# Experts' first product by seven half-size block products, tokens outer in two halves

## The chip, the cores and the metric

One core of a Trainium2 chip. The metric is the time of one execution on the device in microseconds, lower is better. The times below are of one program that computes everything; the host only rearranges inputs and the output.

## What is computed

Three steps on 2176 rows (4 batches of 512 tokens and 32 state rows) of width 512:

```
attention per batch and head: xread = softmax(x s^T / 8) s;  sread = softmax(s x^T / 8) x
dense:    h = x @ w_in (512 x 2048);  g = h - tanh(h);  x = g @ w_out
experts:  P = exp(x @ w_gate - max), 8 rounds of row and column normalisation
          out = sum over e of P[:, e] * (relu(x @ w1[e]) @ w2[e])     8 experts, 512 x 1024 x 512
```

All products of the dense part and of the experts are made to nearly full precision from rounded parts: an operand `a` is split into `a_hi` (rounded to the type float32r, by ScalarE) and `a_lo = a - a_hi`, and a product is `hi*hi + hi*lo + lo*hi`, three matmuls in a faster single-pass type.

## The kernel before, in words

Every engine runs its own program; semaphores order them. Loads and stores are issued by SyncE.

**Attention** (`scores_T`, `transposes1`, `sread` and others) takes some 58 us. **Dense** (`dense`, four passes `hb` over half blocks of the weights) runs for each pass over the state rows (j = 0) and four batches (j = 1 to 4), four blocks of hidden units each, with `up_batch` (6 matmuls), the tanh on ScalarE, `h - tanh` and the split on VectorE, and `down_dense` (12 matmuls) two steps behind. `dense_sum` adds the four output banks to `acc`. In the last pass, ScalarE (`mlp_input`) and GpSimd split the finished batches of `acc` for the experts.

**Experts.** Expert outer, four chunks of 512 tokens inner (`chunk`). In a chunk `up` (L1123) makes one block of 128 hidden units for 512 tokens: 4 blocks of depth x 3 matmuls, each 128 x 128 weights (w1) against 512 tokens, into one of three banks. ScalarE (`hidden_expert`, L538) takes relu out of the bank and rounds it, VectorE (L763) makes the low part from the same bank. `down` (L1133), two blocks behind, takes 128 tokens of the hidden block as the weights and 512 columns of w2: 4 tiles of tokens x 3 matmuls, summed over 8 blocks in banks 0 to 3. After a chunk VectorE (`gated`, L901) multiplies each of the four banks by the gate of its tokens and adds it to `yacc`. In chunk 1 of each expert the 128 state rows are done the other way round (`state_up`, `state_turn`, `state_down`). The weights of the next expert are split in the last chunk (`w1_hi`, `w2_hi` on ScalarE, `w1_lo`, `w2_lo` on VectorE). Between two matmuls of one product nothing waits; waits stand ahead of a block.

**Gates.** In chunk 0 of the first expert `logits` makes x @ w_gate from the split parts, `turn_logits` turns it with 17 small transposes, and in chunks 1 and 2 VectorE (`rows`, `columns`) runs the eight rounds, each with one sum over partitions on GpSimd. Outputs of the first expert are kept without gates until then (`keep`, `gate_kept`).

Of the kernel before, what the change touches and what calls it, by code (L numbers as in the profile page):

```python
# [18 lines left out]
B, H, S, NS, D = 4, 8, 512, 32, 64  # L19
# [3 lines left out]
P = 128  # L23
# [24 lines left out]
EXP_STEP = 6  # L48
ST_CHUNK = 1
GATED_EARLY = 2 * ST  # L50
assert SINKHORN == F


def build(nc, xT_d, xn_d, sT_d, w1_d, w2_d, wg_d, out_d):
# [9 lines left out]
    with ctx:  # L64

        start = (nc.sbuf_base + 63) // 64 * 64
        place = [start]

        def sb(name, shape, dt=f32):
            size = 4  # L70
            for n in shape[1:]:
                size *= n
            at = place[0]
            place[0] += (size + 31) // 32 * 32
            return nc.alloc_sbuf_tensor_at(name, shape, dt, offset=at)


        w1h = sb("w1h", [P, F, KT, P], f32r)
        w1l = sb("w1l", [P, F, KT, P], f32r)
        w2h = sb("w2h", [P, F, DM], f32r)  # L80
        w2l = sb("w2l", [P, F, DM], f32r)
        after_w2l = place[0]


        xh = sb("xh", [P, KT, B * S], f32r)
        xl = sb("xl", [P, KT, B * S], f32r)

        st1 = sb("st1", [P, NST, KT, P])
        st2 = sb("st2", [P, NST, DM])


        shared = place[0]
        acc = sb("acc", [P, KT, T])
        after_acc = place[0]
        place[0] = shared
        yacc = sb("yacc", [P, TQ, DM])
        assert place[0] <= after_acc
        place[0] = after_acc

        hiddens = place[0]  # L100
        hh = sb("hh", [P, NH, S], f32r)
        hl = sb("hl", [P, NH, S], f32r)
        xsh = sb("state_rows_hi", [P, KT, SB], f32r)
        xsl = sb("state_rows_lo", [P, KT, SB], f32r)
        scratch = place[0]


        hs_f = sb("state_hidden", [P, S])
        hsh = sb("state_hidden_T_hi", [P, F, SB], f32r)
        hsl = sb("state_hidden_T_lo", [P, F, SB], f32r)  # L110
        end = place[0]


        place[0] = scratch
        wg = sb("wg", [P, KT, P], f32r)
        wg_raw = sb("wg_raw", [P, KT, E])
        lg_rows = sb("lg_rows", [2 * E, T])
        lg_two = sb("lg_two", [P, TQ, 2 * E])
        end = max(end, place[0])


        place[0] = after_w2l - (F - HF) * DM * 4
        th = sb("tanh_h", [P, S])
        x_st = sb("state_tokens", [P, KT, SB])
        h_st = sb("state_tokens_hidden", [P, NH, SB])
        assert place[0] <= after_w2l

        place[0] = scratch
        sTh = sb("sTh", [P, B // 2, KT, P], f32r)
        sTl = sb("sTl", [P, B // 2, KT, P], f32r)  # L130
        g_h = sb("h_less_tanh", [P, 2, S])
        end = max(end, place[0])

        place[0] = shared
        xT = sb("xT", [P, 2, KT, S])
        xn = sb("xn", [P, 2, ST, DM])
        scT = sb("scT", [P, S])
        assert place[0] <= after_acc

        place[0] = hiddens  # L140

        sT = sb("sT", [P, B // 2, KT, P])
        e2 = sb("e2", [P, 2, S])
        a2T = sb("a2T", [P, ST, P])
        a1 = sb("a1", [P, 2, ST, P])
        nb2 = sb("nb2", [P, G])
        r2 = sb("r2", [P, G])
        m1 = sb("m1", [P, 2, 4 * ST])
        r1 = sb("r1", [P, 2, 4 * ST])
        assert place[0] <= scratch  # L150

        place[0] = end
        ident = sb("ident", [P, P])
        pr = sb("pr", [P, E, TQ])
        gcur = sb("gate_now", [P, TQ])
        rsum = sb("rsum", [P, TQ])
        csum = sb("csum", [P, E])
        call = sb("call", [P, E])
        gmax = sb("gmax", [P, 1])
        amax = sb("amax", [P, 1])  # L160
        assert place[0] <= nc.sbuf_usable_end, (place[0], nc.sbuf_usable_end)
# [7 lines left out]
        lgpsum = bank[7]  # L169
        stpsum = bank[7]  # L170
# [57 lines left out]
        s_x2h = sem("mlp_input_hi")  # L228
        s_x2s = sem("mlp_input_split")
        s_wgin = sem("wgate_loaded")  # L230
        s_wgz = sem("wgate_zeroed")
        s_wgh = sem("wgate_hi_ready")
        s_wg = sem("wgate_split")
        s_lg = sem("logits_ready")
        s_lgc = sem("logits_copied")
        s_lgt = sem("logits_transposed")
        s_lgr = sem("logits_by_token_ready")
# [6 lines left out]
        s_gw = sem("gates_final")  # L244
        s_su = sem("state_rows_hidden_ready")
        s_sr2 = sem("state_rows_relu_ready")
        s_stt = sem("state_rows_transposed")
        s_shi = sem("state_rows_hidden_hi_ready")
        s_shs = sem("state_rows_hidden_split")
# [6 lines left out]

        def own_rows(b, s0=0, s1=S):

            return slice(b * S + s0, b * S + s1)

        def batch(b, s0=0, s1=S):

            return slice(b * TB + s0, b * TB + s1)

        def states(t, k):

            return t[:, k, :].rearrange("p (b n) -> p b n", b=B)[:, :, S:TB]

        def by_batch(t, k):

            return t[:, k, :].rearrange("p (b n) -> p b n", b=B)
# [11 lines left out]


        @block.sync
        def _(sp):
# [19 lines left out]
            def follow_splits(b, more):  # L306

                for i in range(F + 3):
                    if i < F:
                        sp.wait_ge(s_w1, b * F + i + 1)  # L310
                        if i < F - NST:
                            load_w1(b, i + NST)
                        elif more:
                            load_w1(b + 1, i - F + NST)
                    j = i - 3
                    if j >= 0:
                        sp.wait_ge(s_w2, b * F + j + 1)
                        if j < F - NST:
                            load_w2(b, j + NST)
                        elif more:  # L320
                            load_w2(b + 1, j - F + NST)


# [12 lines left out]
            for b in range(2, B):  # L336
                load_x(b)

# [9 lines left out]
            def next_w1(hb, s):  # L348
                sp.wait_ge(s_w1, hb * HF + s + 1)
                sp.dma_start(st1[:, s], w1_d[hb + 1, s]).then_inc(s_w1in[s], 16)  # L350

            def next_w2(hb, s):
                sp.wait_ge(s_w2, hb * HF + s + 1)
                sp.dma_start(st2[:, s], w2_d[hb + 1, s]).then_inc(s_w2in[s], 16)

            for s in range(HF):
                next_w1(DH, s)
            sp.wait_ge(s_m, m_count(DH, 0, 0))
            sp.dma_start(wg_raw[:], wg_d).then_inc(s_wgin, 16)
            for s in range(HF):  # L360
                next_w1(DH + 1, s)
            for f in range(F):
                next_w2(DH + f // HF, f % HF)

            with sp.Fori(DENSE + 1, NB - 1) as b:
                follow_splits(b, True)
            follow_splits(NB - 1, False)

            def store(done, t0, t1):
                sp.wait_ge(s_yfree, ST * (1 + (E - 1) * C) + done)  # L370
                sp.dma_start(out_d[:, t0:t1], yacc[:, t0:t1]).then_inc(s_out, 16)

            store(ST, 0, ST)
            store(2 * ST, ST, 2 * ST)
            sp.wait_ge(s_syf, E)
            sp.dma_start(out_d[:, ST_TILE:TQ], yacc[:, ST_TILE:TQ]).then_inc(s_out, 16)
            store(3 * ST, 2 * ST, 3 * ST)
            for t in range(3 * ST, 4 * ST):
                store(t + 1, t, t + 1)
# [4 lines left out]
        def _(pool):  # L384
# [3 lines left out]
                                    pattern=[[-1, P]], channel_multiplier=1).then_inc(s_ident, 1)  # L388

# [21 lines left out]
            nc.gpsimd.memset(acc[:], 0.0).then_inc(s_acc0, 1)  # L411

            pool.wait_ge(s_m, m_count(DH, 0, 0))
            nc.gpsimd.memset(wg[:].bitcast(f32), 0.0).then_inc(s_wgz, 1)


            for k in range(KT):
                pool.wait_ge(s_x2h, k + 1)
                nc.gpsimd.tensor_tensor(by_batch(xsl, k), states(acc, k), by_batch(xsh, k).bitcast(f32),
                                        ALU.subtract).then_inc(s_x2s, 1)  # L420
            for c in range(C):
                for k in range(KT):
                    pool.wait_ge(s_x2h, (c + 1) * KT + k + 1)
                    nc.gpsimd.tensor_tensor(xl[:, k, own_rows(c)], acc[:, k, batch(c)],
                                            xh[:, k, own_rows(c)].bitcast(f32), ALU.subtract).then_inc(s_x2s, 1)


            pool.wait_ge(s_lmax, 1)
            nc.gpsimd.partition_all_reduce(amax[:], gmax[:], P, RMAX).then_inc(s_amax, 1)
            for r in range(SINKHORN):  # L430
                pool.wait_ge(s_csum, r + 1)
                nc.gpsimd.partition_all_reduce(call[:], csum[:], P, RADD).then_inc(s_call, 1)


        @block.scalar
        def _(act):
# [838 lines left out]
```

## Time and profile before

| | |
|---|---|
| median of 3 runs | 1875.97 us (1874.74 to 1876.88) |
| profiled execution | 1877.22 us, its span 1875.4 us, granted clock 0.997 |
| TensorE, weight loads | 1855.6 us, 1533.4 us, 8409 each |
| VectorE, ScalarE, GpSimd | 615.5, 413.1, 59.9 us |
| read from HBM | 50.61 MB |

The span runs from the first to the last instruction; the profiled execution's own time lies 1.8 us above it. Matmuls overlap in the pipeline, so the mean duration of one (389 ns for 512 columns) is not its interval; that is read from the starts of neighbours. In the rows PE is TensorE, PEld its weight loads, DVE VectorE, ACT ScalarE, POOL GpSimd, and L is a line of the kernel. The type of every TensorE operand is written f32, for float32r too. A product of plain float32 operands leaves two records, each with its own weight load.

### The profile page before, as it was taken

The numbers are of one execution on the slowest core, as the hardware profiler recorded it, in microseconds if no ns is written. First come the engines' busy times: TensorE is split into PE (matmuls) and PEld (weight loads), VectorE is DVE, ScalarE is ACT, GpSimd is POOL, SyncE is SP. The second block draws the span as 40 slices with busy tenths as digits, with TensorE's granted clock in tenths as the row PEclk, the third lists the DMA queues.
The fourth block names the chain that finished last, engine by engine and source line by source line (L and its number), as shares of the span: only waits on it lengthen the run. The fifth ranks groups of instructions, "written<-read, shape, count | busy, mean of one in ns | idle before, by whom it ended". The sixth has DMA issues, their size and how long they took to land.

```text
span 1875.4 us, 20899 instructions
## 1 busy us (share of the span) xinstructions
PE 1855.6 (99%) x8409; PEld 1533.4 (82%) x8409; DVE 615.5 (33%) x1013; ACT 413.1 (22%) x750; POOL 59.9 (3%) x58
## 2 busy tenths in 40 slices
PE   7999999999999999999999999999999999999999
PEld 5888888888888888888888888888888888888887
DVE  6656665621452113211321232123211321142121
ACT  6434344421121112111211121112111211121111
POOL 4200000310000000000000000000000000000000
PEclk9899999999999999999999999999999999999999
DMA  6101101110020002000200020002000200010001
GB/s 230 45 1 45 45 0 51 46 40 1 0 63 29 0 1 63 29 1 0 69 22 1 0 73 18 1 0 74 18 1 0 74 18 1 0 46 23 1 28 45
DMA packets 28231, 56.41 MB, mean 30 GB/s; under 512 B 5104, under 2 KB 5104, under 8 KB 27248
## 3 DMA queue, kind: packets, MB, share of 16 engines
q1 hardware_dynamic: 28144, 55.08, 9.2%
q8 instruction: 76, 1.25, 0.3%
q14 instruction: 11, 0.09, 0.0%
HBM read 50.61 MB, written 4.46 MB: 29 GB/s over the span
## 4 chain that ended last, share of the span: by engine, by line
PE 97%; DVE 1%; issue 1%; ACT 1%; POOL 0%; DVEq 0%; ACTq 0%; POOLq 0%
PE bank L1128 12%; PE bank L1130 12%; PE bank L1129 12%; PE bank L1142 12%; PE bank L1143 12%; PE bank L1144 12%; PE bank L1097 3%; PE bank L1098 3%; PE bank L1099 3%; PE bank L1081 1%; PE bank L1083 1%; PE bank L1082 1%; PE bank L1037 1%; PE bank L1070 1%; PE bank L1173 1%
## 5 line engine op out<-in xcount | busy, mean ns | idle before, releaser
L763 DVE SCALAR_TENSOR_TENSOR hl<-bank,hh 128x512 fp32r<-128x512 f32 x256 | 177.1, 692 | 952.8 <-ACT hh L538 952.8
L1128 PE MATMUL bank<-xh,w1h 128*128 128x512 f32 x1024 | 400.4, 391 | 0.2
L538 ACT ACTIVATE hh<-bank 128x512 fp32r<-128x512 f32 x256 | 153.1, 598 | 1116.2 <-PE bank L1130 1116.2
L1130 PE MATMUL bank<-xh,w1l 128*128 128x512 f32 x1024 | 398.7, 389 | 0.0
L1142 PE MATMUL bank<-w2h,hh 128*128 128x512 f32 x1024 | 398.5, 389 | 0.0
L1129 PE MATMUL bank<-xl,w1h 128*128 128x512 f32 x1024 | 398.5, 389 | 0.0
L1144 PE MATMUL bank<-w2h,hl 128*128 128x512 f32 x1024 | 398.4, 389 | 0.0
L1143 PE MATMUL bank<-w2l,hh 128*128 128x512 f32 x1024 | 398.3, 389 | 0.0
L1128 PEld LDWEIGHTS bank<-xh,w1h 128*128 128x128 f32 x1024 | 192.3, 188 | 40.8 <-issue 1.3
L1130 PEld LDWEIGHTS bank<-xh,w1l 128*128 128x128 f32 x1024 | 192.2, 188 | 40.3
L1142 PEld LDWEIGHTS bank<-w2h,hh 128*128 128x128 f32 x1024 | 192.2, 188 | 40.0
L1144 PEld LDWEIGHTS bank<-w2h,hl 128*128 128x128 f32 x1024 | 192.2, 188 | 39.9
L1143 PEld LDWEIGHTS bank<-w2l,hh 128*128 128x128 f32 x1024 | 192.2, 188 | 39.8
L1129 PEld LDWEIGHTS bank<-xl,w1h 128*128 128x128 f32 x1024 | 192.3, 188 | 39.3
L901 DVE SCALAR_TENSOR_TENSOR yacc<-bank,gate_now,yacc 128x512 f32<-128x512 f32 x112 | 78.1, 751 | 127.2 <-PE bank L1144 127.2
L1097 PE MATMUL bank<-hh,w2h 128*128 128x512 f32 x256 | 100.0, 391 | 0.0
L1098 PE MATMUL bank<-hl,w2h 128*128 128x512 f32 x256 | 99.6, 389 | 0.0
L1099 PE MATMUL bank<-hh,w2l 128*128 128x512 f32 x256 | 99.6, 389 | 0.0
L758 DVE TENSOR_TENSOR hl<-h_less_tanh,hh 128x512 fp32r<-128x512 f32 x64 | 45.3, 708 | 43.9 <-ACT hh L533 43.9
L1097 PEld LDWEIGHTS bank<-hh,w2h 128*128 128x128 f32 x256 | 48.0, 188 | 11.5 <-DVE acc L783 1.2
L533 ACT CAST hh<-h_less_tanh 128x512 fp32r<-128x512 f32 x64 | 39.7, 621 | 79.1 <-DVE h_less_tanh L756 79.1
L1099 PEld LDWEIGHTS bank<-hh,w2l 128*128 128x128 f32 x256 | 48.1, 188 | 10.1
(129 smaller groups left out, 1372.0 us busy)
## 6 DMA issues: line engine op xcount, KB each, us to landing
st<-w SPq DMA_DIRECT2D x160, 256.0 KB, 2.7
xT<-xT SPq DMA_DIRECT2D x8, 512.0 KB, 8.0
xn<-xn SPq DMA_DIRECT2D x4, 1024.0 KB, 6.0
out<-yacc SPq DMA_DIRECT2D x3, 1024.0 KB, 3.9
out<-yacc SPq DMA_DIRECT2D x5, 256.0 KB, 2.1
sT<-sT SPq DMA_DIRECT2D x2, 128.0 KB, 3.3
wg_raw<-wg SPq DMA_DIRECT2D x1, 16.0 KB, 2.4
```

The costliest lines, as they stand in the source:

```text
L538: nc.scalar.activation(hh[:, f % NH], hpsum[f % NH][:], ACT.Relu).then_inc(s_hh, 1)
L763: v.scalar_tensor_tensor(hl[:, f % NH], hpsum[f % NH][:], 0.0, hh[:, f % NH].bitcast(f32), ALU.max, ALU.subtract).then_inc(s_hs, 1)
L901: v.scalar_tensor_tensor(yacc[:, i], ypsum[t][:], gcur[:, i:i + 1], yacc[:, i], ALU.mult, ALU.add).then_inc(s_yfree, 1)
L1097: mm(out, w2h[:, s, at], high, start=(s == 0), stop=False)
L1098: mm(out, w2h[:, s, at], hl[:, i % NH, :], start=False, stop=False)
L1099: last = mm(out, w2l[:, s, at], high, start=False, stop=(s == HF - 1))
L1128: mm(out, w1h[:, f, k, :], xh[:, k, own_rows(c)], start=(k == 0), stop=False)
L1129: mm(out, w1h[:, f, k, :], xl[:, k, own_rows(c)], start=False, stop=False)
L1130: last = mm(out, w1l[:, f, k, :], xh[:, k, own_rows(c)], start=False, stop=(k == KT - 1))
L1142: mm(out, hh[:, f % NH, at], w2h[:, f], start=(f == 0), stop=False)
L1143: mm(out, hh[:, f % NH, at], w2l[:, f], start=False, stop=False)
L1144: last = mm(out, hl[:, f % NH, at], w2h[:, f], start=False, stop=(f == F - 1))
```

## The change

The loop is turned: all 16 half experts ("units" of 512 hidden units) for chunks 0 and 1, then the 16 again for chunks 2 and 3. A unit with two chunks is a visit of four stages: chunk, then pair `p` of hidden blocks. Each stage (`stage`) computes two hidden blocks for 512 tokens. Depth (512), hidden (256) and tokens (512) are each cut in two, and the 2 x 2 x 2 block product is made with seven products of 128 hidden units x 256 tokens x 256 deep, the form of Strassen and Winograd: seven factors of tokens and seven of weights, three of them plain blocks and four sums. The products are combined on VectorE into the hidden blocks, from PSUM and SBUF. Sums and low parts of all factors are made on GpSimd, high parts on ScalarE. The token factors of two chunks are resident; those of chunks 2 and 3 replace them at the turn of the halves. Outputs are drained every second stage, since a unit is half an expert. Logits are made from the unsplit `acc` with 32-column products in plain float32 and a small selecting product in place of the transposes. The state rows use plain blocks and one sum, 24 matmuls of 256 columns a unit, in the first half only.

TensorE's new program:

```diff
+            def product(which, u, cc, p):
+                out = {P1: apsum[:, 0:HT], P2: apsum[:, HT:S], P6: bpsum[:, 0:HT], P7: bpsum[:, HT:S],
+                       P4: cpsum[:, 0:HT], P5: cpsum[:, HT:S], P3: bpsum[:, 0:HT]}[which]
+                a, b = FACTORS[which]
+                w, xs, xr = wc[u], xch[cc], xcl[cc]
+                for k in range(HK):
+                    mm(out, w[:, p, 0, b, k, :], xs[:, a, k, :], start=(k == 0), stop=False)
+                    mm(out, w[:, p, 0, b, k, :], xr[:, a, k, :], start=False, stop=False)
+                    last = mm(out, w[:, p, 1, b, k, :], xs[:, a, k, :], start=False, stop=(k == HK - 1))
+                last.then_inc(s_p, 1)
+            def stage(x, l, half):
+                n, u, part, cc, p = 8 * x + l, l // 4, l % 4, l // 2 % 2, l % 2
...
+                if cc == 0:
+                    pe.wait_ge(s_wfs, 3 * (2 * vis + p + 1))
+                if half and part == 2:
+                    pe.wait_ge(s_xfs, 16)
+                if not first:
+                    pe.wait_ge(s_h11, n)
+                product(P1, u, cc, p)
+                product(P2, u, cc, p)
+                if not first:
+                    pe.wait_ge(s_h12, n)
+                product(P6, u, cc, p)
+                product(P7, u, cc, p)
+                if not first:
+                    pe.wait_ge(s_v, n)
+                product(P4, u, cc, p)
+                product(P5, u, cc, p)
...
+                if not first:
+                    down_even(*before)
+                pe.wait_ge(s_u3, n + 1)
+                product(P3, u, cc, p)
+                if first:
+                    turn_logits()
+                else:
+                    down_odd(*before)
...
+            pe.wait_ge(s_xfs, 8)
+            for l in range(8):
+                stage(0, l, 0)
+            with pe.Fori(1, E) as x:
+                for l in range(8):
+                    stage(x, l, 0)
+            pe.wait_ge(s_xfs, 12)
+            with pe.Fori(E, 2 * E) as x:
+                for l in range(8):
+                    stage(x, l, 1)
+            down_even(2 * E - 1, 7)
+            down_odd(2 * E - 1, 7)
```

`down_even` and `down_odd` hold 12 matmuls each, of the form of `down`, for the stage before. State rows: `state_up` (18 matmuls) after part 1, `state_up_even` (6) and `state_turn` in part 2, `state_down` (12) in part 3. VectorE's stage:

```diff
+                sum2(n)
+                hidden11(x, l)
+                sum3(n)
+                hidden_late(x, l)
+                sum25(n)
+                lo11(n, p)
...
+                lo_late(n, p)
+                hidden12(n, p)
+                lo12(n, p)
...
+                if l % 2 == 0 and not first:
+                    outputs(q, c, how)
...
+            def sum2(n):
+                dve.wait_ge(s_p, OPS * n + P7)
+                dve.wait_ge(s_c1, n + 1)
+                v.tensor_tensor(u2[:], bpsum[:, 0:HT], prod1[:], ALU.add).then_inc(s_u2, 1)
+            def hidden11(x, l):
+                v.tensor_tensor(hf[l % 2][:, 0, 0:HT], apsum[:, HT:S], prod1[:], ALU.add).then_inc(s_h11, 1)
+            def sum3(n):
+                dve.wait_ge(s_h11, n + 1)
+                v.tensor_tensor(u3[:], bpsum[:, HT:S], u2[:], ALU.add).then_inc(s_u3, 1)
+            def sum25(n):
+                v.tensor_tensor(u2[:], cpsum[:, HT:S], u2[:], ALU.add).then_inc(s_v, 1)
+            def hidden_late(x, l):
+                v.tensor_tensor(hf[p][:, :, HT:S], cpsum[:].rearrange("p (f n) -> p f n", f=2),
+                                u3[:].unsqueeze(1).broadcast_to([P, 2, HT]), ALU.add).then_inc(s_late, 1)
+            def lo11(n, p):
+                v.scalar_tensor_tensor(rl[p][:, 0, 0:HT], hf[p][:, 0, 0:HT], 0.0, raw(rh[p][:, 0, 0:HT]),
+                                       ALU.max, ALU.subtract).then_inc(s_l11, 1)
+            def hidden12(n, p):
+                dve.wait_ge(s_p, OPS * n + P3)
+                v.tensor_tensor(hf[p][:, 1, 0:HT], bpsum[:, 0:HT], u2[:], ALU.add).then_inc(s_h12, 1)
```

`lo_late` (2 x 256 columns) and `lo12` have the form of `lo11`. ScalarE's stage is `copy1` (P1 to SBUF), two `w2_hi` in parts 0 and 1, `relu11`, `relu_late`, `relu12`, then the high parts of the next unit's w1 factors. At the turn of the halves, and for chunk 3 two stages on:

```diff
+            expert(E - 1, 0, {6: (late_plain_hi, 2), 7: (token_sums_hi, 2)})
+            expert(E, 1, {0: (late_plain_hi, 3), 1: (token_sums_hi, 3)})
```

GpSimd's program of a visit, and of the token factors:

```diff
+            def visit(v, u, more=True, late=None):
+                w2_lo(v, 0)
+                w2_lo(v, 1)
+                if late == 3:
+                    token_sums(3)
+                if more:
+                    w1_pair_sums(v + 1, 1 - u, 0)
+                w2_lo(v, 2)
+                w2_lo(v, 3)
+                if late == 3:
+                    token_lo(3)
+                if more:
+                    w1_pair_lo(v + 1, 1 - u, 0)
+                if more:
+                    w1_pair_sums(v + 1, 1 - u, 1)
+                if late == 2:
+                    token_sums(2)
+                    token_lo(2)
+                if more:
+                    w1_pair_lo(v + 1, 1 - u, 1)
```

`token_sums` is four sums of 512 columns, `token_lo` three low parts of 512 and one of 2048, after ScalarE's high parts of the same sizes; `w1_pair_sums` four of 256, `w1_pair_lo` low parts of 512, 256 and 1024. SyncE loads unit v once the pair, or the w2 block, of unit v - 1 in its place is split.

Gates: the rounds `rows` and `columns` are spread over stages 2 to 8, one at the end of a stage, and in stages 5, 7 and 8 one in its middle; GpSimd's sums over partitions stand at fixed places among its splits. Logits:

```diff
+            def logits():
+                pe.wait_ge(s_wgin, 16)
+                pe.wait_ge(s_dsum, DENSE_SUMS)
+                for b in [B] + list(range(B)):
+                    src, n = (acc_s[:], SB) if b == B else (acc[:, b], S)
+                    out = lgpsum if b == B else bank[b]
+                    for k in range(KT):
+                        at = slice(k * LG, (k + 1) * LG)
+                        last = mm(out[at, 0:n], wg[:, k, :], src[:, k, :], start=True, stop=True)
+                    last.then_inc(s_lg, 1)
```

In the last dense pass the splits of w1 and w2 and the copies of `mlp_input` are left out; in their place ScalarE has the high parts of the factors of chunks 0 and 1 and of the first weight pair, GpSimd the sums and low parts.

## Rows read from the trace of the kernel before

**Rows 1.** The page, part 1: busy us (share of the span) x instructions
```profile
PE 1855.6 (99%) x8409; PEld 1533.4 (82%) x8409; DVE 615.5 (33%) x1013; ACT 413.1 (22%) x750; POOL 59.9 (3%) x58
```

**Rows 2.** The page, part 4: shares of the chain that ended last
```profile
PE 97%; DVE 1%; issue 1%; ACT 1%; POOL 0%; DVEq 0%; ACTq 0%; POOLq 0%
```

**Rows 3.** Windows, one expert: length, PE, PEld, DVE, ACT, POOL, clock, DMA
```profile
610.00:796.00 186.00, 186.00 (x826) 153.92 (x825) 44.93 (x68) 29.72 (x52) 0.00 (x0) 1.00 0.08 23
```

**Rows 4.** Timeline of TensorE inside a product: start us, duration us, instruction
```profile
899.95 0.39 PE L1128 MATMUL bank<-xh,w1h 128*128 128x512 f32 x1
...
903.58 0.39 PE L1129 MATMUL bank<-xl,w1h 128*128 128x512 f32 x1
```

**Rows 5.** Timeline of TensorE, 128 columns: seven starts, then the next product
```profile
413.99 0.28 PE L1209 MATMUL bank<-state_rows_lo,wg 128*128 128x128 f32 x1
...
414.77 0.45 PE L1128 MATMUL bank<-xh,w1h 128*128 128x512 f32 x1
```

**Rows 6.** Chain in order of time, four-byte products: start, us, what, records
```profile
139.06 2.68 PE bank L1070 x24
```

**Rows 7.** Groups of VectorE by form: busy us, mean ns | idle before
```profile
L901 DVE SCALAR_TENSOR_TENSOR yacc<-bank,gate_now,yacc 128x512 f32<-128x512 f32 x112 | 78.1, 751 | 127.2 <-PE bank L1144 127.2
L756 DVE TENSOR_TENSOR h_less_tanh<-bank,tanh_h 128x512 f32<-128x512 f32 x64 | 43.9, 686 | 35.1 <-ACT tanh_h L531 34.7
L750 DVE TENSOR_TENSOR state_tokens_hidden<-bank,tanh_h 128x128 f32<-128x128 f32 x16 | 4.6, 286 | 3.5 <-ACT tanh_h L523 3.5
```

**Rows 8.** Groups of ScalarE by form
```profile
L538 ACT ACTIVATE hh<-bank 128x512 fp32r<-128x512 f32 x256 | 153.1, 598 | 1116.2 <-PE bank L1130 1116.2
L523 ACT ACTIVATE tanh_h<-bank 128x128 f32<-128x128 f32 x16 | 4.4, 278 | 25.6 <-PE bank L1070 23.9 <-DVE state_tokens_hidden L750 1.0
L495 ACT CAST sTh<-sT 128x1024 fp32r<-128x1024 f32 x1 | 1.0, 1030 | 0.0
```

**Rows 9.** Groups of GpSimd by form
```profile
L402 POOL TENSOR_TENSOR a<-a,r 128x512 f32<-128x512 f32 x8 | 8.4, 1050 | 6.6 <-DVE r L703 6.6
L406 POOL TENSOR_TENSOR sTl<-sT,sTh 128x1024 fp32r<-128x1024 f32 x1 | 2.4, 2354 | 0.0
```

**Rows 10.** The page, part 6: weight loads, KB each, us to landing
```profile
st<-w SPq DMA_DIRECT2D x160, 256.0 KB, 2.7
```

**Rows 11.** Timelines of GpSimd and VectorE in the last dense pass
```profile
333.35 5.57 POOL L424 TENSOR_TENSOR xl<-acc,xh 128x512 fp32r<-128x512 f32 x4 [11.28 <-ACT xh L619]
335.36 0.69 DVE L756 TENSOR_TENSOR h_less_tanh<-bank,tanh_h 128x512 f32<-128x512 f32 x1 [1.80 <-ACT tanh_h L531]
337.70 1.77 DVE L810 TENSOR_TENSOR w1l<-st,w1h 128x512 fp32r<-128x512 f32 x1
```

**Rows 12.** Timeline of VectorE: dense outputs of chunks 0 and 1 added
```profile
327.90 2.48 DVE L783 TENSOR_TENSOR acc<-bank,acc 128x512 f32<-128x512 f32 x4
344.22 2.48 DVE L783 TENSOR_TENSOR acc<-bank,acc 128x512 f32<-128x512 f32 x4
```

**Rows 13.** Timeline of TensorE: the experts' first matmul
```profile
374.04 0.39 PE L1128 MATMUL bank<-xh,w1h 128*128 128x512 f32 x1
```

**Rows 14.** Timeline of TensorE: turned logits, and two score products
```profile
36.20 1.08 PE L983 MATMUL bank<-xT,sT 128*64 128x512 f32 x4
420.42 1.22 PE L1216 MATMUL bank<-ident,lg_rows 16*128 16x16 f32 x17
```

**Rows 15.** Timeline of TensorE, a wait, and the window behind it
```profile
51.33 1.11 PE L1011 MATMUL bank<-ident,a 128*128 128x128 f32 x4 [0.97 <-POOL a L402]
51.00:61.00 10.00, 9.68 (x40) 9.09 (x41) 4.49 (x8) 4.67 (x10) 4.18 (x2) 0.50 0.00 0
```

**Rows 16.** Groups of weight loads by form
```profile
L1129 PEld LDWEIGHTS bank<-xl,w1h 128*128 128x128 f32 x1024 | 192.3, 188 | 39.3
```

More of the change, by code:

```diff
@@ L103, in build @@
[L103 to L118, printed above, removed]
@@ L163, in ps @@
+        assert end <= nc.sbuf_usable_end, (end, nc.sbuf_usable_end)
+        th = hs_f
+        prod1 = u3
+        gmax, amax = most[:, 0:1], most[:, 1:2]
         def ps(name, shape):
@@ new lines, in token_lo @@
+            def token_lo(c):
+                hi, lo = xch[c % 2], xcl[c % 2]
+                pool.wait_ge(s_xfh, 4 * c + 2)
+                for k in range(2):
+                    less(lo[:, A11 + k], tokens(c, k * HK, False), raw(hi[:, A11 + k]), s_xfs)
+                pool.wait_ge(s_xfh, 4 * c + 3)
+                less(lo[:, A22], tokens(c, HK, True), raw(hi[:, A22]), s_xfs)
+                pool.wait_ge(s_xfh, 4 * c + 4)
+                less(lo[:, S1:OPS], xf[c % 2][:, S1:OPS], raw(hi[:, S1:OPS]), s_xfs)
@@ new lines, in _ @@
+            token_lo(0)
+            state_rows_lo()
+            token_sums(1)
+            token_lo(1)
+            for p in range(2):
+                w1_pair_sums(0, 0, p)
+                w1_pair_lo(0, 0, p)
+            w2_lo(0, 0)
+            w2_lo(0, 1)
+            w1_pair_sums(1, 1, 0)
+            max_of_all()
+            w2_lo(0, 2)
+            w2_lo(0, 3)
+            w1_pair_lo(1, 1, 0)
+            w1_pair_sums(1, 1, 1)
+            sums_of_all(0)
+            w1_pair_lo(1, 1, 1)
@@ L562, in dense @@
                         m_hi(hb, 1, s)
-                    if j == 2:
+                    if j == 2 and not last:
                         w1_half_hi(hb + 1, s)
@@ new lines, in expert, with exponentials @@
+            def expert(x, half, extra={}, last=False):
+                for l in range(8):
+                    stage(x, l, half, extra.get(l), not (last and l >= 4))
+            def logits():
+                act.wait_ge(s_lg, B + 1)
+                nc.scalar.copy(hs_f[:, 0:SB], lgpsum[:, 0:SB]).then_inc(s_lgc, 1)
+                for b in range(B):
+                    nc.scalar.copy(lg_rows[:, b], bank[b][:]).then_inc(s_lgc, 1)
+            def exponentials(c):
+                act.wait_ge(s_shift, 1)
+                nc.scalar.activation(pr[:], pr[:], ACT.Exp, bias=amax).then_inc(s_exp, 1)
@@ L798, in dense @@
                         m_lo(hb, 1, s)
-                    if j == 2:
+                    if j == 2 and not last:
                         w1_half_lo(hb + 1, s)
@@ L802, in dense @@
                         m_lo(hb + 1, 0, s)
-                    if j == 3 and last:
-                        w1_lo(DENSE, HF + s)
-                w2_half_lo(hb + 1, 0)
+                if not last:
+                    w2_half_lo(hb + 1, 0)
                 dense_sum(hb, DC - 1)
@@ new lines, in keep_tokens @@
+            def keep_tokens(c):
+                for t in range(ST):
+                    gate_kept(c * ST + t)
+            dve.wait_ge(s_ident, 1)
+            own(v.reduce_sum(sel[:], ident[:].rearrange("p (k e) -> p e k", k=KT)[:, 0:E], X_AX))
+            dve.sem_inc(s_sel, 1)
+            stage(0, 0, 0, end=logits_max)
+            stage(0, 1, 0, end=logits_shift)
+            dve.wait_ge(s_xfs, 8)
+            stage(0, 2, 0, "keep", end=lambda: rows(0))
+            stage(0, 3, 0, states="keep", end=lambda: round_after(1))
@@ new lines, in _ @@
+            stage(1, 2, 0, end=lambda: keep_tokens(1))
+            for l in range(3, 8):
+                stage(1, l, 0)
+            with dve.Fori(2, E) as x:
+                expert(x, 0)
+            stage(E, 0, 1, end=lambda: own_gate(E, 1))
+            stage(E, 1, 1)
+            dve.wait_ge(s_xfs, 12)
+            stage(E, 2, 1, "first")
+            stage(E, 3, 1)
+            dve.wait_ge(s_xfs, 16)
+            stage(E, 4, 1, "first")
+            for l in range(5, 8):
+                stage(E, l, 1)
@@ L970, in _ @@
+            with dve.Fori(E + 1, 2 * E) as x:
+                expert(x, 1)
+            outputs(8 * E - 1, 3, "gated")
         @block.tensor
@@ new lines, in down_even, with down_odd, state_columns @@
+            def down_even(x, l):
+                n = 8 * x + l
+                pe.wait_ge(s_l11, n + 1)
+                down_tiles(x, l, 0, (0, 1))
+                pe.wait_ge(s_llate, n + 1)
+                down_tiles(x, l, 0, (2, 3))
+            def down_odd(x, l):
+                n, p, vis = 8 * x + l, l % 2, 2 * x + l // 4
+                down_tiles(x, l, 1, (2, 3))
+                pe.wait_ge(s_l12, n + 1)
+                down_tiles(x, l, 1, (0, 1))
+            def state_columns(at, b, u, k0, opens, closes):
+                out = stpsum[:, at * HT:(at + 1) * HT]
+                for k in range(HK):
+                    mm(out, xsh[:, k0 + k, :], wc[u][:, :, 0, b, k, :], start=opens and k == 0, stop=False)
+                    mm(out, xsh[:, k0 + k, :], wc[u][:, :, 1, b, k, :], start=False, stop=False)
+                    last = mm(out, xsl[:, k0 + k, :], wc[u][:, :, 0, b, k, :], start=False, stop=closes and k == HK - 1)
+                return last
```

921 lines of the change are left out of this document (506 added, 415 removed).

## The prediction

> **What bounds the kernel now.** I read the busy shares first, then the chain of waits, then one expert in the windows view, then single instructions. TensorE is busy 99% of the span [rows 1], and the chain that ended last is TensorE for 97% [rows 2]. In one expert's 186 us it is busy for all of them at full clock, while VectorE works 45 us, ScalarE 30 and GpSimd nothing [rows 3]. So time can only come out of TensorE's own stream, and the other engines have room. In that stream a 128x512 product starts every 0.2269 us (16 intervals in 3.63 us) [rows 4]; 512 columns at the full 2.4 GHz would be 0.2133, so each carries 13.4 ns on top.
>
> **First product: what is removed and added.** An expert has 4 chunks x 8 blocks x 12 first products of 512 columns plus 24 for the state rows: 408, or 3264 over 8 experts, 3264 x 0.2269 = 740.6 us. Now a stage (two blocks of 128 hidden units, 512 tokens) runs 7 products x 6 matmuls of 256 columns. Stages: 16 units x 8 = 128, so 5376 matmuls, and the state rows take 4 x 6 per unit, 16 units in the first half: 384. Together 5760, each half as wide. The second product (24 of 512 columns a stage) keeps its count, 3072, as do the state rows' 192 and their 64 transposes.
>
> The whole change hangs on the interval T of a 256-column matmul with its own weight load, which the trace does not show. Neighbours: with 128 columns in the same type the interval is 0.78/7 = 111.4 ns, where the stream alone would be 53, so something other than the columns, by all likelihood the load, sets it [rows 5]. Four-byte products run as two records each; 24 such records take 2.68 us, 111.7 ns each, again 128 columns [rows 6]. Nothing faster is seen, so 111.7 is the lower end. For the upper end the 13.4 ns could be a fixed cost of each matmul: 106.7 + 13.4 = 120. If it goes with the columns, T is half of 226.9, 113.4. Two of these three rows lie at 111 to 113, so I take 115, and keep 120 as a rival. 5760 x 0.115 = 662.4, a gain of 78.2 us; at 111.7 it is 97.2, at 120 it is 49.4. At 0.1237 the gain would just pay for the 28 us of costs below (740.6 - 28 = 712.6; / 5760).
>
> The Trainium skill, "TensorE: Matmul & The Clock Gate", section "Back-to-back issue gap", gives columns / 2.4 + 2.5 ns for a warm matmul, 109.2 ns here; by that the gain would be 111.6 us. This case's trace disagrees at 512 columns (226.9 ns against 215.8), so I give it no weight beyond the lower end.
>
> **Does the combination keep up?** A stage on TensorE is 42 x 0.115 + 24 x 0.2269 = 10.28 us (10.9 before). From the stage's start: P1, P2, P6, P7 end at 2.8, P4 and P5 at 4.1, `down_even` at 6.9, P3 at 7.6, `down_odd` at 10.3. Interpolating 128 and 512 columns, VectorE needs 0.42 us for 256 (0.286 and 0.686) and ScalarE 0.39 (0.278 and 0.598) [rows 7, 8]. P3 waits for `sum3`: sum2, hidden11, sum3 from 3.0 end by 4.3, against 6.9: slack 2.6. P6 of the next stage waits for hidden12: P3 ends at 7.6, hidden12 by 8.2, wanted at 11.7. Even stages then drain four output banks (0.751 each, started 0.68 apart): `lo12` by 9.1, banks until about 11.9, next `sum2` at 13.2. VectorE's work: seven of 0.42 and two of 0.69, in all 4.3 us, and 3.0 of banks every second stage: 5.8 of 10.3. In the first half a unit's four stages also carry the state rows, 5.8 us more on TensorE against some 2.3 on VectorE. ScalarE about 3 a stage. I cost the steady stages at no wait; the cover that hides them is the four products and `down_even` ahead of P3.
>
> GpSimd now splits all weights. It takes 2.35 us for 1024 columns into the rounded type, and 1.05 for 512 plain ones [rows 9]. Per unit: four w2 blocks 4.8, eight sums of 256 columns 4.8, lows 2 x (1.2 + 0.6 + 2.35) = 8.3: about 18 us of 41. Its last low waits for ScalarE's third stage and ends near 33 us, eight ahead of need. The experts' weights are fetched twice, 64 MB where 32; a 256 KB block lands in 2.7 us [rows 10] and four a stage are wanted in 10: hidden.
>
> **GpSimd against VectorE.** While GpSimd worked on four splits (5.57 us), a VectorE instruction with two operands in SBUF took 1.77 us, where one reading PSUM stayed at 0.69 [rows 11]. Three of the stage's nine (`lo11`, `lo_late`, `lo12`) are of the slow kind, and a GpSimd instruction of 2.35 us is longer than those it collided with. Within the slack above (a `sum2` may start 5 us after `lo12`'s place) this costs nothing in steady stages; where it does not fit it is the rival below.
>
> The Trainium skill, "SBUF — State Buffer", section "Who interferes with whom", says that a VectorE instruction with two SBUF inputs and a GpSimd one that reads SBUF exclude each other and the loser blocks. The row agrees: 1.77 is 0.68 plus most of a 1.4 us split.
>
> **End of the dense part.** Chunk 0 of the dense output is complete at 330.4, chunk 1 at 346.7 [rows 12], and experts began at 374.04 [rows 13]. GpSimd now has for both chunks four sums (1.05 each) and lows of 3584 columns (8.4 us), the state rows and the first weight pair. Followed in order, with ScalarE's casts (1.03 for 1024 columns [rows 8], so 1.9 for 2048): lows of chunk 0 at 347, state rows 348.5, sums of chunk 1 at 353, its lows 363.5, the pair's lows 371.6. That is 2.4 ahead of 374. But its 4.6 us instructions block VectorE's `hl` split, which has some 2.7 us before TensorE waits. Bounds 0 and 8 us; I take 3.
>
> **Logits and gates.** Out: 32 matmuls of 512 (7.3), 8 of 128 (0.9), 17 turns (1.2) [rows 14]: 9.4. In: 16 four-byte products 32 columns wide of 512 tokens. Four records, or two products 64 wide, took about 1.0 [rows 14]: 0.5 each, 8 us; 4 if four groups of columns run at once, 13.7 if one by one in four passes. I take 6, plus states 0.9, 17 turns of two records at 0.1117 = 3.8, and 1.5 of waiting for copies: 12.2, so +3 (bounds 0 and +10). The gate rounds (2.3 us of VectorE, partly two SBUF operands) now stand in stages that already hold 6 us, and each asks an answer of a busy GpSimd: 0 to 12 us, I take 4.
>
> **The two changes of token factors.** This is where I see TensorE wait. Before the second half it waits for chunk 2 (`s_xfs` 12). ScalarE casts the sums after `relu12` of the last stage (with its state rows 13.0 us long; relu12 ends at 11.2), so at 13.1, and GpSimd then needs 4.6 for 2048 columns: 17.7, a wait of 4.7. Two stages on it waits for chunk 3 (`s_xfs` 16): relu12 8.6, two weight casts 2, the sums' cast 1.9, GpSimd 4.6: 17.1 against 10.3, 6.8. And the clock: after a wait of 0.97 us (with one like it just before) the granted clock stood at 0.50, the 1.2 GHz level, for 51 to 61 us, with the engine busy 9.68 of 10 [rows 15]; such a stretch costs up to 5. I take 3 for each: 17.5 together, bounds 5 and 25. The last drain and store keep their form.
>
> **Sum.** The profiled execution's own time is 1877.2 (span 1875.4 and 1.8 around it), 1.2 above the median of 1876.0. 1877.2 - 78.2 + 3 + 3 + 4 + 17.5 = 1826.5.
>
> **Rivals.**
> - *The 13.4 ns is fixed per matmul*, T = 120: 5760 x 5 ns = 28.8 more, 1855. For it: no row shows a cost that shrinks with the columns. Against it: 106.7 ns of passes in the two-record products fit into 111.7.
> - *GpSimd's lock sets the stage* (the other side). If each of the 18 to 22 us GpSimd works in a unit blocks VectorE, a stage costs VectorE 5.8 + 5.5 = 11.3 us, 1.0 over TensorE: 128 us, 1955. It decides once blocking exceeds 4.5 us a stage, and turns the change slower from 0.4 us of wait a stage (50 us). For it: 1.77 against 0.68. Against: only three short instructions can be hit, and GpSimd idles half the unit.
> - *The load sets the interval.* Its record is 188 ns [rows 16]; with T = 188 the 5760 take 1083 us, 2248 in all. Against it: the 111 ns rows hold the same loads.
> - *Little is lost outside the stream*: T = 112 and no waits at the factors: 1877 - 95.5 + 8 = 1790.
>
> **Chances.** Forecast 0.53 (own range 1805 to 1850), fixed cost 0.26, lock 0.09, load 0.04, little lost 0.08. The range for 8 in 10 takes in the second case: 1796 to 1862. Faster by over 0.2% (3.7 us, about what a measurement of this kernel tells from no change) needs less than 1872: 0.88; within it 0.02; slower 0.10.
>
> **What would show it.** In the profile after: a T of 113 to 117 ns between 256-column starts inside a product, and no idle time of TensorE before P3 (right), or P3 waiting for `sum3` (lock). Two gaps of 4 to 7 us ahead of the second half and two stages on, with clock 0.5 behind them. `lo` instructions with a longer mean than 0.42 while `sum2` keeps it. The forecast is wrong if T is over 0.1237, or if waits in the repeated stages sum to over 30 us.

## The result, and the profile after

The changed kernel takes 1895.3 us (1892.9 to 1896.0, 4 runs), the kernel before 1876.4 in the same job: a ratio of 1.010, 95% interval 1.0083 to 1.0118: slower by 1.0%, where the forecast, 1826.5, was faster by 2.7%. The profiled execution has a span of 1891.1 us and an own time of 1892.9.

The page after, parts 1, 2 (the lines of TensorE and of its clock) and 4, the answers to [rows 1, 2]:

```profile
PE 1824.1 (96%) x10922; PEld 1619.8 (86%) x10922; DVE 1057.9 (56%) x1953; ACT 609.5 (32%) x1193; POOL 744.5 (39%) x648
...
PE   7999999996699999999999999799999999999999
...
PEclk9999999998899999999999999999999999999999
...
PE 90%; issue 3%; POOL 3%; DVE 2%; ACT 1%; DMA 0%; SPq 0%; POOLq 0%; DVEq 0%; ACTq 0%
```

TensorE fell from 99% to 96% and its share of the chain from 97% to 90%. The tenth and eleventh slice (425 to 520 us) have it at 6 tenths with the clock at 8. The windows view has two stretches of repeated stages, then the one with the loss (columns as in [rows 3]):

```profile
600.00:1100.00 500.00, 500.00 (x3157) 453.70 (x3156) 264.78 (x502) 144.01 (x290) 205.34 (x181) 1.00 0.14 43
1300.00:1800.00 500.00, 500.00 (x3139) 453.47 (x3138) 289.66 (x528) 153.43 (x309) 241.16 (x212) 1.00 0.16 50
424.00:600.00 176.00, 140.94 (x824) 126.48 (x823) 90.47 (x198) 37.68 (x77) 63.60 (x61) 0.88 0.11 37
438.00:530.00 92.00, 57.01 (x283) 50.02 (x282) 33.37 (x93) 12.72 (x26) 22.03 (x24) 0.78 0.08 23
```

In the repeated stages TensorE is never idle and runs at full clock. Between 438 and 530 it is idle for 35 us, and a mean clock of 0.78 is (1 - 0.78) / 0.5 x 92 = 40 us at the 1.2 GHz level, part of them inside the waits. This is where the rounds of the gates' normalisation stand. Behind one of the waits:

```profile
451.40 0.28 PE L1378 MATMUL bank<-token_factors_hi,w_factors 128*128 128x256 f32 x1
455.48 0.58 PE L1376 MATMUL bank<-token_factors_hi,w_factors 128*128 128x256 f32 x1 [3.80 <-DVE hidden L985]
...
456.08 0.42 PE L1378 MATMUL bank<-token_factors_hi,w_factors 128*128 128x256 f32 x1
...
460.56 0.41 PE L1378 MATMUL bank<-token_factors_hi,w_factors 128*128 128x256 f32 x1
```

After it 21 intervals take 4.48 us, 0.213 each; ahead of it the starts lie 0.12 apart. TensorE's waits, by what it waited for (us in total, times, longest):

```profile
PE bank L1376 <- POOL token_factors_lo L410: 11.3, 2, 6.4
PE bank L1420 <- DVE state_hidden L1002: 10.5, 1, 10.5
PE bank L1376 <- DVE hidden L985: 10.0, 2, 6.2
PE bank L1376 <- DVE sum L961: 9.7, 1, 9.7
...
PE bank L1343 <- DVE acc L1025: 3.3, 2, 1.7
PE bank L1454 <- DVE state_hidden_T_lo L1012: 3.1, 1, 3.1
```

The first line is the forecast's two changes of token factors. The three `state_hidden`, `hidden` and `sum` lines and the last are waits for VectorE, and VectorE waited in its own order for GpSimd's sum over the partitions. All those waits in one line (us in total, times, longest), then two of them:

```profile
DVE call L1083 <- POOL call L484: 52.2, 5, 13.3
...
452.16 0.17 DVE L1083 TENSOR_SCALAR call<-call 128x8 f32<-128x8 f32 x1 [10.34 <-POOL call L484]
...
468.77 0.17 DVE L1083 TENSOR_SCALAR call<-call 128x8 f32<-128x8 f32 x1 [12.44 <-POOL call L484]
```

GpSimd, all that it did from 449 to 492 us:

```profile
451.70 0.43 POOL L484 PARTITION_ALL_REDUCE call<-csum  x1 [5.82 <-issue]
459.69 2.49 POOL L410 TENSOR_TENSOR w2l<-st,w2h 128x512 fp32r<-128x512 f32 x2 [7.56 <-PE bank L1378]
468.31 0.43 POOL L484 PARTITION_ALL_REDUCE call<-csum  x1 [6.14 <-issue]
475.78 1.43 POOL L410 TENSOR_TENSOR w_sums<-st 128x256 f32<-128x256 f32 x2 [7.04 <-issue]
477.17 1.54 POOL L410 TENSOR_TENSOR w_sums<-st,w_sums 128x256 f32<-128x256 f32 x2
484.54 0.43 POOL L484 PARTITION_ALL_REDUCE call<-csum  x1 [5.83 <-issue]
491.90 1.28 POOL L410 TENSOR_TENSOR w_factors<-st,w_factors 128x512 fp32r<-128x512 f32 x1 [6.93 <-issue]
```

GpSimd is not busy here: it stands still for 5.8 to 6.1 us ahead of each reduction that follows a plain instruction, and for 6.9 to 7.6 ahead of each plain instruction that follows a reduction, nearly always with "issue", nothing that the profile shows, as the cause. The kernel before had its eight reductions one behind the other.

### The profile page after: what moved, and what is told of

Same layout as the page of the kernel before. It is cut to its first block, busy times and chain, and to the rows that moved or that the text cites. A ratio compares the mean times of both kernels' runs of the same rounds, so it can differ in the third digit from the quotient of the medians.

```text
span 1891.1 us, 30690 instructions
## 1 busy us (share of the span) xinstructions
PE 1824.1 (96%) x10922; PEld 1619.8 (86%) x10922; DVE 1057.9 (56%) x1953; ACT 609.5 (32%) x1193; POOL 744.5 (39%) x648
## 4 chain that ended last, share of the span: by engine, by line
PE 90%; issue 3%; POOL 3%; DVE 2%; ACT 1%; DMA 0%; SPq 0%; POOLq 0%; DVEq 0%; ACTq 0%
PE bank L1393 12%; PE bank L1394 12%; PE bank L1395 12%; PE bank L1376 11%; PE bank L1378 11%; PE bank L1377 11%; PE bank L1343 3%; PE bank L1344 3%; PE bank L1345 3%; PE bank L1329 1%; PE bank L1328 1%; PE bank L1327 1%; PE bank L1283 1%; PE bank L1422 1%; PE bank L1421 1%
## 5 line engine op out<-in xcount | busy, mean ns | idle before, releaser
L1376 PE MATMUL bank<-token_factors_hi,w_factors 128*128 128x256 f32 x1792 | 513.9, 287 | 31.0 <-POOL token_factors_lo L410 11.3
L1378 PE MATMUL bank<-token_factors_hi,w_factors 128*128 128x256 f32 x1792 | 512.5, 286 | 0.0
L1377 PE MATMUL bank<-token_factors_lo,w_factors 128*128 128x256 f32 x1792 | 512.3, 286 | 0.0
L1393 PE MATMUL bank<-w2h,relu_hi 128*128 128x512 f32 x1024 | 403.4, 394 | 1.8 <-issue 1.8
L1394 PE MATMUL bank<-w2l,relu_hi 128*128 128x512 f32 x1024 | 402.9, 393 | 0.0
L1395 PE MATMUL bank<-w2h,relu_lo 128*128 128x512 f32 x1024 | 399.6, 390 | 0.0
L1376 PEld LDWEIGHTS bank<-token_factors_hi,w_factors 128*128 128x128 f32 x1792 | 348.2, 194 | 42.4 <-DVE sum L961 10.6
L1377 PEld LDWEIGHTS bank<-token_factors_lo,w_factors 128*128 128x128 f32 x1792 | 348.3, 194 | 8.5
L1378 PEld LDWEIGHTS bank<-token_factors_hi,w_factors 128*128 128x128 f32 x1792 | 348.0, 194 | 0.0
L1395 PEld LDWEIGHTS bank<-w2h,relu_lo 128*128 128x128 f32 x1024 | 193.4, 189 | 42.1
L1393 PEld LDWEIGHTS bank<-w2h,relu_hi 128*128 128x128 f32 x1024 | 194.2, 190 | 35.7 <-issue 2.0
L1394 PEld LDWEIGHTS bank<-w2l,relu_hi 128*128 128x128 f32 x1024 | 194.2, 190 | 31.2
```

What stands on the lines that cost most here:

```text
L1376: mm(out, w[:, p, 0, b, k, :], xs[:, a, k, :], start=(k == 0), stop=False)
L1377: mm(out, w[:, p, 0, b, k, :], xr[:, a, k, :], start=False, stop=False)
L1378: last = mm(out, w[:, p, 1, b, k, :], xs[:, a, k, :], start=False, stop=(k == HK - 1))
L1393: mm(out, rh[p][:, j, at], w2h[:, f], start=(f == 0), stop=False)
L1394: mm(out, rh[p][:, j, at], w2l[:, f], start=False, stop=False)
L1395: last = mm(out, rl[p][:, j, at], w2h[:, f], start=False, stop=(f == HF - 1))
```

## The experiments

Theory A was that this change-over costs the time in the gates' rounds. The rivals: B, the rounds only stand in the wrong places of VectorE's order; C, the shared port lets GpSimd slow VectorE in the repeated stages. Beside them stood one more question, the interval T of the matmuls, which came out at 120 ns and not 115. Baselines of the three jobs: 1876.8, 1876.5 and 1876.6 us.

**No sum over the partitions.** The changed kernel with a plain instruction in place of the reduction (left out: the sum over the partitions, so the gates' values differ).

```diff
-nc.gpsimd.partition_all_reduce(call[:], csum[:], P, RADD).then_inc(s_call, 1)
+nc.gpsimd.tensor_tensor(call[:], csum[:], csum[:], ALU.add).then_inc(s_call, 1)
```

> The changed kernel, but the eight sums over partitions of the gate rounds are left out: GpSimd doubles the column sums with a plain tensor instruction at the same place, so waits and their order stay. The gates are then not the reference's. Theory A (GpSimd pays 6 to 7 us, with no instruction shown, each time it changes between the reduction over partitions and plain tensor instructions; VectorE waits for it in order, TensorE for VectorE): the six gaps of TensorE at 440 to 525 us, 37 us in all, and most of the half-clock stretches behind them go, 1845 to 1860. Theory B (the rounds' own work on VectorE and the collisions of its two-input instructions with GpSimd fill the stages): VectorE's work and GpSimd's splits are unchanged, so at most 5 us less, 1890.

Measured: 1849.0 us, ratio 0.9855 (0.9839 to 0.9872), 46.3 us less than the changed kernel. The order of the work, its waits and GpSimd's other work are the same, so B falls. GpSimd's trace shows the standstill gone where the two instructions are of one kind:

```profile
438.87 0.20 POOL L484 TENSOR_TENSOR call<-csum 128x8 f32<-128x8 f32 x1 [5.34 <-DVE csum L1079]
439.02 2.55 POOL L410 TENSOR_TENSOR w2l<-st,w2h 128x512 fp32r<-128x512 f32 x2
```

**The sum on TensorE.** The same sum, kept, as one product by a matrix of ones (`wg`, no longer needed, is filled with them); each round has a stage of its own, ending in its late part.

```diff
-            sums_of_all(0)
...
+                if isinstance(n, int) and 3 <= n < 3 + SINKHORN:
...
+                    pe.wait_ge(s_csum, n - 2)
+                    mm(apsum[:, 0:E], wg[:].rearrange("p k l -> p (k l)"), csum[:], start=True, stop=True).then_inc(s_call, 1)
```

> The changed kernel with the sums over partitions made by TensorE (a 128x128 matrix of ones against the 8 columns, into the free half bank ahead of P3), one round a stage in stages 3 to 10. The maximum stays on GpSimd. The result is the reference's. Theory A: 1845 to 1860, as with the sums left out, since a small matmul costs 0.2 us. Theory B: 1890, since the same rounds stand in the same stages.

Measured: 1849.3 us, ratio 0.9857 (0.9841 to 0.9874). Its windows row for the stretch of the loss:

```profile
424.00:600.00 176.00, 175.70 (x1125) 159.90 (x1124) 110.29 (x238) 51.98 (x106) 79.91 (x71) 1.00 0.15 46
```

301 more matmuls in the same 176 us, at full clock; at 66 in a stage of 10.48 us that is 47.8 us. The eight products are in it for nothing that can be seen. Since this edit also moves the rounds in VectorE's order, it is the run before that rules B out; this one shows that the sum itself can be had without the loss.

**The kernel before, with the change-over put in.** One instruction of 128x1 on GpSimd between its reductions.

```diff
+if r:
+    nc.gpsimd.tensor_tensor(gmax[:], gmax[:], gmax[:], ALU.add)
 nc.gpsimd.partition_all_reduce(call[:], csum[:], P, RADD).then_inc(s_call, 1)
```

> The kernel before, with one tensor_tensor of a single column put on GpSimd ahead of the second to the eighth sum over the partitions, work of under 0.1 us each. Theory A (each passage between the reduction and a plain tensor instruction makes GpSimd idle for 6 to 7.5 us, whatever the kernel): some 13 us more for each of seven rounds, which follow each other at 5.4 us in the kernel before, with VectorE waiting in order for each; 91 us of waits, of which a half or more reaches TensorE: 1915 to 1970 us, with idle of 6 to 7 us put down to issue ahead of both kinds of instruction. Theory B (in the changed kernel the rounds only stand behind other GpSimd work and in the wrong places of VectorE's order): no change, 1875 to 1879 us.

Measured: 1929.5 us, ratio 1.0285 (1.0268 to 1.0302): 53 us for seven instructions of 0.18 us. GpSimd in it, and in the second fence the first two reductions of the kernel before:

```profile
486.61 0.44 POOL L434 PARTITION_ALL_REDUCE call<-csum  x1 [33.07 <-DVE csum L840]
493.76 0.18 POOL L433 TENSOR_TENSOR gmax<-gmax 128x1 f32<-128x1 f32 x1 [6.71 <-issue]
499.71 0.43 POOL L434 PARTITION_ALL_REDUCE call<-csum  x1 [5.77 <-issue]
506.92 0.18 POOL L433 TENSOR_TENSOR gmax<-gmax 128x1 f32<-128x1 f32 x1 [6.78 <-issue]
513.26 0.43 POOL L434 PARTITION_ALL_REDUCE call<-csum  x1 [6.16 <-issue]
```

```profile
488.33 0.44 POOL L432 PARTITION_ALL_REDUCE call<-csum  x1 [33.07 <-DVE csum L838]
491.80 0.40 POOL L432 PARTITION_ALL_REDUCE call<-csum  x1 [3.03 <-DVE csum L838]
```

From one reduction to the next it is 13.1 to 14.0 us over the seven, where the kernel before has 2.9 to 5.4, set by VectorE's next `csum`; from the first to the last 95.3 us against 33.4, 61.9 more. With this A is shown in both directions and in both kernels: for a pair of change-overs GpSimd stands still for 12.5 to 13.4 us here and 12.8 to 13.9 in the changed kernel, whatever stands between, and the 53 us are what of the 61.9 passed through VectorE's order to TensorE (five waits for `hl`, 40.5 us in all and the longest 12.2, and half clock behind them).

The Trainium skill, "GPSIMD Engine Reference", section "2.1 Instruction dispatch", says that the first call to a freshly loaded GpSimd kernel pays a load of about 6 us, with no instruction in the profile to show it. The rows agree on size and on the missing record (5.77 to 6.16 us ahead of a reduction). They add that this was not paid once: it came back at each alternation, and the way back cost 6.7 to 7.5. That the standstill is this load no run here shows.

**Less of GpSimd's other work.** The changed kernel with the low parts of w2 and of w1's plain blocks cut to 8 of 128 columns (w2: of 512) from the third unit on (left out: the rest of those low parts, which keep stale values). In `visit`, `z` is `slice(0, 8)`.

```diff
-less(w2l[:, f], st2[:, f], raw(w2h[:, f]), s_w2)
+less(w2l[:, f, z], st2[:, f, z], raw(w2h[:, f, z]), s_w2)
...
-less(lo[:, B22], st1[:, 2 * p + 1, HK:KT], raw(hi[:, B22]), s_wfs)
+less(lo[:, B22, :, z], st1[:, 2 * p + 1, HK:KT, z], raw(hi[:, B22, :, z]), s_wfs)
...
```

> The changed kernel with GpSimd's low parts of both weight matrices cut to 8 of 128 (or of 512) columns in the units from the third on, 9 of its 18 us in each 42 us of a steady unit (left out: those products are computed with stale low parts). Theory C (the shared port: GpSimd's instructions slow VectorE's, and with them TensorE, in the repeated stages): several tens of us less, down to 1850. Theory A (the repeated stages run at TensorE's rate whatever GpSimd does, and the loss is in the gate's rounds and at the half turn): 1889 to 1896 us, at most 6 us less, at the half turn, where GpSimd's work stands ahead of the new token factors.

Measured: 1894.0 us, ratio 1.0097 (1.0080 to 1.0114), not to be told from the changed kernel. GpSimd's work between 600 and 1100 us fell from 205.3 to 124.8 us, by two fifths. One form of VectorE between 600 and 1100 us, in the changed kernel and in this one:

```profile
L978 DVE SCALAR_TENSOR_TENSOR relu_lo<-hidden,relu_hi 128x256 fp32r<-128x256 f32 x41 | 27.9, 681 | 0.0
```

```profile
L978 DVE SCALAR_TENSOR_TENSOR relu_lo<-hidden,relu_hi 128x256 fp32r<-128x256 f32 x41 | 17.1, 416 | 0.0
```

The collision is real, 0.27 us on each of these, and cost nothing, since TensorE had no idle time for it to lengthen: C falls.

**New token factors one stage earlier.** ScalarE casts the token sums in the stage ahead and some weight factors a stage later, and GpSimd makes chunk 3's factors first.

```diff
-expert(E - 1, 0, {6: (late_plain_hi, 2), 7: (token_sums_hi, 2)})
-expert(E, 1, {0: (late_plain_hi, 3), 1: (token_sums_hi, 3)})
+expert(E - 1, 0, {6: (both_hi, 2)})
+expert(E, 1, {0: (both_hi, 3)}, shift=True)
```

> The changed kernel with ScalarE's casts of the token sums one stage earlier at the turn of the halves, and GpSimd making the factors of chunk 3 ahead of the next unit's weight factors. Both theories: the two waits of 5.3 and 6.75 us for token factors and the 10.2 us at half clock behind them go, 12 + 5 = 17 us less, 1878. If GpSimd's queue is what is full there, the waits only move to the weight factors: 1890.

Measured: 1879.1 us, ratio 1.0015 (1.0006 to 1.0025), 16.2 less than the changed kernel; TensorE no longer waits for `token_factors_lo`.

**Both.** The TensorE sum and the earlier factors together.

> Both of the edits that won time apart: the rounds' sums over the partitions as a matmul by ones on TensorE, and the token factors of the second half made one stage earlier. If the two losses are at separate places and nothing takes their place, their gains add: 1849.3 - 16.2 = 1833 us (1830 to 1837), a ratio of 0.977 to the kernel before. If what one freed had been hiding the other, it stays nearer 1849.

Measured: 1833.4 us, ratio 0.9772 (0.9756 to 0.9789). The gains add to 0.3 us (46.0 + 16.2 = 62.2; found 61.9), and this version beats both kernels. Its page:

```profile
PE 1811.1 (99%) x10938; PEld 1610.0 (88%) x10938; DVE 1064.3 (58%) x1954; ACT 609.2 (33%) x1193; POOL 744.1 (41%) x640
```

**Width alone.** Two runs of the kernel before, its first product cut into narrower matmuls with the same columns in sum, 3072 of them more: `cols` is 256 + 256 columns in the first run, 384 + 128 in the second.

```diff
-                for k in range(KT):
-                    mm(out, w1h[:, f, k, :], xh[:, k, own_rows(c)], start=(k == 0), stop=False)
...
+                for h in range(2):
...
+                    for k in range(KT):
+                        mm(out[:, cols], w1h[:, f, k, :], xh[:, k, at], start=(k == 0), stop=False)
...
```

> The kernel before with each matmul of the experts' first product cut into two of 256 columns, 6144 for 3072, nothing else changed. If the 13.4 ns above the columns are fixed per matmul: 3072 more of them, 41 us, 1917. If they go with the columns (T = 113.4): no change, 1876. At T = 115: 10 us, 1886.

Measured: 1921.0 us, ratio 1.0239 (1.0222 to 1.0256): 44.2 us for 3072 matmuls, 14.4 ns each. TensorE inside one of its products:

```profile
700.05 0.28 PE L1132 MATMUL bank<-xh,w1l 128*128 128x256 f32 x1
700.17 0.28 PE L1130 MATMUL bank<-xh,w1h 128*128 128x256 f32 x1
700.29 0.28 PE L1131 MATMUL bank<-xl,w1h 128*128 128x256 f32 x1
```

> The kernel before, with each of the 3072 first products of 512 token columns cut into one of 384 and one of 128 columns (the even cut gave 1921 us). Theory F (every matmul costs its columns at 2.4 GHz and 13.3 ns, nothing else): 160 + 13.3 and 53.3 + 13.3 ns, 240 in all as with the even cut: 1921 us. Theory G (besides the 13.3 ns there is a floor of some 111 ns under a matmul with its own weight load, which is what the rows of 128 columns showed and from which I took 115 for 256 columns): 173.3 + 111.7 = 285 ns, 58 more than before for each of 3072, 179 us: 2056 us.

Measured: 2066.2 us, ratio 1.1012 (1.0993 to 1.1030): 189.6 us, 61.7 ns for each pair against 58 by theory G and 13.3 by F. TensorE in it, ten intervals of each width:

```profile
703.97 0.34 PE L1132 MATMUL bank<-xl,w1h 128*128 128x384 f32 x1
...
705.74 0.33 PE L1133 MATMUL bank<-xh,w1l 128*128 128x384 f32 x1
...
705.97 0.27 PE L1132 MATMUL bank<-xl,w1h 128*128 128x128 f32 x1
...
707.08 0.28 PE L1133 MATMUL bank<-xh,w1l 128*128 128x128 f32 x1
```

That is 177 ns at 384 columns and 111 at 128, together the 288 that the run's time gives (226.7 + 61.7). So there are two terms: a part on top of the columns that does not shrink with them (226.7 - 213.3 = 13.4 ns at 512 columns, 177 - 160 = 17 at 384, 120.0 - 106.7 = 13.3 at 256), and a floor near 111 ns that decides at 128 columns and no longer at 256. That the floor is the weight load is not shown.

## Why the prediction was wrong

Two steps failed: the gate rounds were put at 4 us and cost 46.0, which made a faster kernel a slower one, and the interval T was put at 115 ns and is 120, another 28.8 us. By the prediction's own steps, from the profiled own time of before, 1877.2:

- **The stream, T = 115.** Mis-sized. Inside a product of the changed kernel the starts lie 0.12 us apart:

```profile
700.11 0.28 PE L1376 MATMUL bank<-token_factors_hi,w_factors 128*128 128x256 f32 x1
700.23 0.28 PE L1377 MATMUL bank<-token_factors_lo,w_factors 128*128 128x256 f32 x1
700.35 0.28 PE L1378 MATMUL bank<-token_factors_hi,w_factors 128*128 128x256 f32 x1
```

  The gain was 49.4 us and not 78.2: 28.8 lost, exactly the rival with the fixed cost (0.26 of the chances). I took the value between two rows at 111 ns, but those were at 128 columns and show the floor, which the last run separates from the fixed part. The one row that could be scaled to 256 columns was the 512-column one, and its excess of 13.4 ns had to be carried over whole or halved; I mixed it with a row of another regime.
- **Repeated stages at no wait.** Right. 500.00 of 500.00 us busy, twice; taking two fifths of GpSimd's work there away gained nothing.
- **GpSimd against VectorE.** Right in both parts: the collision is there (681 against 416 ns) and free in repeated stages.
- **End of the dense part, 3.** Right: two waits of 1.65 us before L1343, starts 2.04 us apart where 0.23 is usual, 3.6 in all.
- **Logits, +3.** Somewhat too dear. TensorE in the changed kernel, and its window behind the second line:

```profile
377.62 3.62 PE L1509 MATMUL bank<-acc,wg 128*32 128x512 f32 x32
...
382.12 3.72 PE L1523 MATMUL bank<-sel,lg_rows 128*128 128x8 f32 x32
...
387.00:389.00 2.00, 2.00 (x12) 2.00 (x11) 0.00 (x0) 0.64 (x2) 0.09 (x1) 0.50 0.00 0
```

  With the state rows 3.8 and 3.7 us. Behind the products of 8 columns the granted clock stood at 0.50, though TensorE had not been idle: the next fifteen intervals took 3.21 us where 1.80 is usual, 1.4 more. With 0.4 at the seams that is 9.3, against 9.4 removed: -0.1. The 16 logits products of 512 columns left 32 records in 3.62 us, 113 ns each, so groups of 32 output columns ran side by side, as in my bound of 4.
- **The two changes of token factors, 17.5.** Right in place and nearly in size. The waits are 4.89 and 6.36 us (4.7 and 6.8 expected). The stretches at half clock behind them cost 1.4 and 2.2 by TensorE's starts, where I took 3 each. Putting both aside gained 16.2:

```profile
1198.82 0.58 PE L1376 MATMUL bank<-token_factors_hi,w_factors 128*128 128x256 f32 x1 [4.89 <-POOL token_factors_lo L410]
...
1227.80 0.58 PE L1376 MATMUL bank<-token_factors_hi,w_factors 128*128 128x256 f32 x1 [6.36 <-POOL token_factors_lo L410]
```

- **The gate rounds, 4 (bounds 0 and 12).** This is the step that turned the result: "each asks an answer of a busy GpSimd". I priced GpSimd's answer by its work, a queue of 1 to 2 us instructions, and not by the change of kind between the two. It cost 46.0 us by the run with the sum on TensorE, 46.3 by the one without the sum. Even my upper bound left it out, because no row of before had a plain instruction right behind a reduction or close ahead of one that was due; the place to look was there, though: GpSimd's order in the changed code alternates the two kinds, which the old one never did.

The sum with the measured terms: 1877.2 - 49.4 + 0 + 3.6 - 0.1 + 46.0 + 16.2 = 1893.5, against 1892.9 of the profiled execution. That execution is the fastest of its four; from median to median the same terms give 1892.7 against 1895.3, and without the last two 1830.6 against the 1833.4 of the version with both edits. So some 2.7 us stay open. Of the difference to the forecast, 42 us are the gate rounds, 28.8 the interval, and -3.8 the other three. Without the gate rounds' loss the change would have been faster (1849), as the run with the sum on TensorE is.

How the gate rounds' loss divides can be read from the two windows of 424 to 600 us: TensorE was idle for 35.1 us in the changed kernel and 0.3 with the sum on TensorE. Of the 47.8 us, then, 34.8 are waits, and the other 13 went to the lower clock, at which a matmul of 256 columns takes 213 ns and not 120. What inside GpSimd the change-over consists of stays open.

## What to carry to other kernels

Look in GpSimd's order for a reduction over the partitions between plain tensor instructions: count some 13 us of GpSimd's time for each such pair (46 us for the eight sums here, 53 for seven pairs in the kernel before, reached the kernel's time), and if an engine waits for it in order, put the sum on TensorE by a matrix of ones or keep the reductions together. When a product is traded for fewer but narrower matmuls, charge the excess of a wide one over its columns to every matmul in full, and check that a narrow neighbour row is not at its floor. Seven products for eight would have been an eighth of the chunks' first products, 87 us of 697 (3072 x 0.2269); at 120 ns for half the columns 52 of them came (5376 x 0.120 = 645).

## What was not expected of the hardware

- GpSimd: 5.8 to 6.6 us ahead of a partition reduction that follows a plain instruction, 6.7 to 7.6 the other way, at every alternation, with "issue" as the only trace of it; back to back, reductions start 2.9 to 5.4 us apart, when VectorE's next sums are ready.
- TensorE: 120.0 ns between starts at 256 columns and 226.7 at 512, both some 13.3 over their columns; at 1.2 GHz the same 256 columns start every 0.213 us, which is the columns alone. The part on top is seen at the full clock only.
- TensorE's clock fell to 0.50 without a wait: behind 3.7 us of products of 8 columns it stood there from 387 to 389 us.
- Plain float32 products with 32 output columns each, in four groups: their records started every 113 ns on average at 512 token columns, half the interval of a float32r matmul of 512 (226.7).
